# Old-state products, one chunk's scaling and the prologue's finishes of y in a fused attention and two-FFN kernel, put elsewhere

## The reference

```python
for t in range(S):
    cur = einsum('bhd,bhe->bhde', u[None] * kt, vt)
    y[:, :, t] = einsum('bhd,bhde->bhe', rt, state + cur)
    state = wt[:, :, :, None] * state + einsum('bhd,bhe->bhde', kt, vt)
x = y as (tokens, heads * channels)
h = x @ w_in;  x = where(h > 0, h, exp(min(h, 0)) - 1) @ w_out
out = sum over e of p[:, e:e+1] * (maximum(x @ w1[e], 0) @ w2[e])
```

## Time and profile before

| | |
|---|---|
| median of 3 runs | 698.22 us (696.87 to 699.43) |
| the profiled execution | 699.0 us, of which 696.8 are the span |
| TensorE matmuls busy | 99% of the span |
| VectorE busy | 38% |
| ScalarE busy | 26% |
| GpSimd busy | 23% |
| mean granted TensorE clock | 0.988 |

### The profile page before, as it was taken

One profiled execution on the slowest core, in us unless ns is written; L12 is line 12 of the kernel. 1 busy time (PEld: TensorE's weight loads), 2 busy tenths in 40 slices (PEclk: granted clock), 3 DMA queues, 4 the chain that ended last, 5 costly groups with the idle time before them and its releaser, 6 DMA issues.

```text
span 696.8 us, 10225 instructions
## 1 busy us (share of the span) xinstructions
PE 687.2 (99%) x3971; PEld 608.8 (87%) x3971; DVE 263.1 (38%) x471; ACT 181.3 (26%) x339; POOL 162.6 (23%) x181
## 2 busy tenths in 40 slices
PE   8989999999999999999999999999999999999998
PEld 6879999988878888899999999999999999999997
DVE  7568766675543433312131212121212121212122
ACT  3653443343343544411111111111111111111110
POOL 3899113110100366610005600006500000000000
PEclk9989999999999999999999999999999999999999
DMA  9902332220000232200002300003200000001011
GB/s 341 406 34 82 125 115 81 81 81 1 1 1 0 69 91 90 92 24 1 1 0 91 91 1 0 0 23 91 69 1 0 0 0 1 1 1 45 0 45 46
DMA packets 12854, 38.70 MB, mean 56 GB/s; under 512 B 1552, under 2 KB 3344, under 8 KB 12816
## 3 DMA queue, kind: packets, MB, share of 16 engines
q1 hardware_dynamic: 12528, 37.77, 15.9%
q10 hardware_dynamic: 288, 0.39, 0.2%
HBM read 35.80 MB, written 2.36 MB: 55 GB/s over the span
## 4 chain that ended last, share of the span: by engine, by line
PE 95%; DVE 3%; issue 1%; ACT 1%; DMA 0%; DVEq 0%
PE bank L852 29%; PE bank L854 29%; PE bank L853 28%; PE bank L804 3%; PE bank L760 2%; PE bank L800 1%; PE bank L815 1%; PE bank L771 1%; PE bank L784 1%; DVE w_lo L597 1%; DVE fr L514 1%; DVE bank L629 0%; DMA rkw<-rkw_dram 0%; PE bank L826 0%; DVE att L552 0%
## 5 line engine op out<-in xcount | busy, mean ns | idle before, releaser
L852 PE MATMUL bank<-x_lo,w_hi 128*128 128x512 f32 (+2 forms) x480 | 183.1, 382 | 1.2 <-DVE g_lo L635 0.9
L702 DVE SCALAR_TENSOR_TENSOR g_lo<-bank,g_hi 128x512 fp32r<-128x512 f32 x96 | 66.4, 691 | 308.5 <-ACT g_hi L482 308.5
L854 PE MATMUL bank<-x_hi,w_hi 128*128 128x512 f32 (+2 forms) x480 | 179.6, 374 | 0.0
L853 PE MATMUL bank<-x_hi,w_lo 128*128 128x512 f32 (+2 forms) x480 | 178.4, 372 | 0.0
L482 ACT ACTIVATE g_hi<-bank 128x512 fp32r<-128x512 f32 x96 | 57.5, 599 | 340.9 <-PE bank L854 340.9
L854 PE MATMUL bank<-w_hi,g_hi 128*128 128x384 f32 x384 | 129.7, 338 | 0.0
L853 PE MATMUL bank<-w_hi,g_lo 128*128 128x384 f32 x384 | 129.6, 337 | 0.0
L852 PE MATMUL bank<-w_lo,g_hi 128*128 128x384 f32 x384 | 129.3, 337 | 0.0
L854 PEld LDWEIGHTS bank<-x_hi,w_hi 128*128 128x128 f32 x480 | 91.1, 190 | 17.5
L852 PEld LDWEIGHTS bank<-x_lo,w_hi 128*128 128x128 f32 x480 | 91.1, 190 | 15.0 <-DVE g_lo L635 2.1
L853 PEld LDWEIGHTS bank<-x_hi,w_lo 128*128 128x128 f32 x480 | 91.4, 190 | 12.7
(11 more groups left out here) (67 smaller groups left out, 570.2 us busy)
## 6 DMA issues: line engine op xcount, KB each, us to landing
raw<-w_dram SPq DMA_DIRECT2D x48, 384.0 KB, 3.1
rkw<-rkw_dram SPq DMA_DIRECT2D x10, 772.5 KB, 4.4
tok<-tok_dram SPq DMA_DIRECT2D x12, 576.0 KB, 4.2
out_dram<-acc SPq DMA_DIRECT2D x10, 192.0 KB, 1.9
rkw<-rkw_dram SPq DMA_DIRECT2D x2, 512.0 KB, 4.5
rkw<-rkw_dram SPq DMA_DIRECT2D x2, 260.5 KB, 3.5
out_dram<-acc ACTq DMA_DIRECT2D x2, 192.0 KB, 1.9
u_rep<-u_dram SPq DMA_DIRECT2D x1, 192.0 KB, 6.2
```

The costliest lines, as they stand in the source:

```text
L702: dve.scalar_tensor_tensor(out=g2[1][:, r, :], in0=p_h[j % 2][:, :], scalar=0.0, in1=g2[0][:, r, :].bitcast(F32), op0=ALU.max, op1=ALU.sub ...
L852: pe.matmul(out, wh, ml, start=start, stop=False)
L853: pe.matmul(out, wl, mh, start=False, stop=False)
L854: return pe.matmul(out, wh, mh, start=False, stop=stop)
```

## The change

Four edits. `values` is cut in two: `old_values(c)` issues the sixteen products with the old state (and takes the waits for masks and state), and TensorE calls it two steps behind the scores, between `up(n)` and `down1(n - LAG)`; the products with the masked scores stay at the end of that step. The second half of the mask moves ahead of `elu`, next to the first. A second table, `SCALED`, equals `SCORES` but for chunk 2, whose entry is 6 instead of 7, and the scaling of k and r (`products`, `inverses`, `scale_k`, `scale_r`) follows it; `scale_state` does not. In the prologue, VectorE's second half of `lo_w(0)` goes behind both `finish_y`, and TensorE's single fill between the two turns of y goes behind them, to make four.

```diff
--- before.py
+++ after.py
@@ -65,6 +65,8 @@
 FIRST = TILES[0][1] // CH
 
 SCORES = {c: 4 * c - 1 for c in range(FIRST, NC)}
+
+SCALED = {c: step - (c == FIRST) for c, step in SCORES.items()}
 NUPDATE = NC - B
 LO_VECTOR = (0, 3, 5)
 LO_POOL = (1, 2, 4, 6, 7, 8, 9, 10, 11, 12, 13, 14, 15)
@@ -239,9 +241,9 @@
         def halves(ap):
             return ap.rearrange("p (a h i) -> p a h i", h=2, i=HALF)
 
-        def due(n, offset):
-
-            return [c for c, step in SCORES.items() if step + offset == n]
+        def due(n, offset, steps=SCORES):
+
+            return [c for c, step in steps.items() if step + offset == n]
 
         def rk_done(c):
             return 3 + 4 * (c - 1)
@@ -616,9 +618,9 @@
             mask_scores(1, 1, BANKS1)
             bonus(1)
             lo_w(0, 0)
-            lo_w(0, 1)
             finish_y(0, BANKS0)
             finish_y(1, BANKS1)
+            lo_w(0, 1)
             lo_x(0, BANKS0["yt"])
             lo_x(1, BANKS1["yt"])
 
@@ -659,6 +661,7 @@
             for n in range(STEP1):
                 for c in due(n, 1):
                     mask_scores(c, 0, BESIDE)
+                    mask_scores(c, 1, BESIDE)
                 for c in due(n, 3):
                     finish_y(c, BESIDE)
                 for c in due(n, 4):
@@ -668,8 +671,6 @@
                 elu(n)
                 for c in due(n, 0):
                     bonus(c)
-                for c in due(n, 1):
-                    mask_scores(c, 1, BESIDE)
                 for c in due(n, -1):
                     scale_state(c)
                 if n == 0:
@@ -685,12 +686,12 @@
                 if n in LO_AFTER:
                     lo_w(LO_AFTER[n], 0)
                     lo_w(LO_AFTER[n], 1)
-                for c in due(n, -3):
+                for c in due(n, -3, SCALED):
                     products(c)
-                for c in due(n, -2):
+                for c in due(n, -2, SCALED):
                     inverses(c)
                     scale_k(c)
-                for c in due(n, -1):
+                for c in due(n, -1, SCALED):
                     scale_r(c)
                 if n == STEP1 - J1 + 4:
                     normalise_probs()
@@ -786,23 +787,26 @@
                                         start=True, stop=True)
                 ins.then_inc(s_pu, 1)
 
+            def old_values(c, banks):
+
+                pe.wait_ge(s_att, c * 2 + 2)
+                pe.wait_ge(s_st, c - 1)
+                q = q_of(c)
+                for h in range(H):
+                    p, o = h // 2, h % 2
+                    rows = slice(64 * o, 64 * o + D)
+                    pe.matmul(banks["y"][o][:, p * D:(p + 1) * D], q[rows, p * CH:(p + 1) * CH],
+                              st[rows, c % 2, p, :], start=h < 2, stop=False, skip_group_check=True)
+
             def values(c, banks):
 
                 landed(pe, s_tok, c)
                 pe.wait_ge(s_att, c * 2 + 2)
-                q, v = q_of(c), v_of(c)
-                old = c >= FIRST
-                if old:
-                    pe.wait_ge(s_st, c - 1)
-                    for h in range(H):
-                        p, o = h // 2, h % 2
-                        rows = slice(64 * o, 64 * o + D)
-                        pe.matmul(banks["y"][o][:, p * D:(p + 1) * D], q[rows, p * CH:(p + 1) * CH],
-                                  st[rows, c % 2, p, :], start=h < 2, stop=False, skip_group_check=True)
+                v = v_of(c)
                 for h in range(H):
                     p, o = h // 2, h % 2
                     ins = pe.matmul(banks["y"][o][:, p * D:(p + 1) * D], att[:, o, p, :],
-                                    v[:, h * D:(h + 1) * D], start=not old and h == 0, stop=True,
+                                    v[:, h * D:(h + 1) * D], start=c < FIRST and h == 0, stop=True,
                                     skip_group_check=True)
                 ins.then_inc(s_py, 1)
 
@@ -841,9 +845,8 @@
             fill(1, 2)
             values(1, BANKS1)
             turn_y(0, BANKS0)
-            fill(1, 1)
             turn_y(1, BANKS1)
-            fill(3, 1)
+            fill(4, 1)
 
 
             def passes(out, w_parts, m_parts, start, stop):
@@ -897,6 +900,8 @@
                 if t == 0:
                     slice_ready(pe, j)
                 up(p_h[n % 2][:, 0:width(n)], tokens(t), j)
+                for c in due(n, 2):
+                    old_values(c, BESIDE)
                 if n >= LAG:
                     down1(n - LAG)
                 if n == 1:
```

## The result

Over eight runs the changed kernel has a median of 693.12 us (692.98 to 693.66), the kernel before 698.39 us (694.61 to 699.43) on the same chips: ratio 0.9934, 95% interval 0.9917 to 0.9952. That is 5.3 us less. As striking is the spread, 0.7 us against 4.8.

A forecast was written before the change was run, and what follows sets the result against it. TensorE, busy 687.2 of 696.8 us, was taken as the bound, with its stops and low clock. 0.75 + 2.2 + 2.96 - 1.6 = 4.3 off 699.0 gives 694.7, less 0.4 for run scatter: 694.3 us, range 692.4 to 697.3.

The forecast's parts named there:

- first rival: The stop ahead of step 7 brings no clock fall, full clock through step 7: 692.8 us, chance 0.28.
- The prologue: VectorE's second low half of slice 0 behind both finishes of y, first expansion sooner: 0.75 us won, bounds 0 and 1.0.
- The new stop: Chunk 2's earlier scaling: some 2.05 us stop ahead of step 7, short clock fall behind it; 2.2 us won.
- The split's gain: Old-state products between expansion and contraction: no clock falls behind the values, 2.96 us won, ends 0 and 2.96.
- The split's price: Extra change between wide and small matmuls, 0.16 us a chunk: 1.6 us lost over ten, ends 0 and 3.2.
- GpSimd: POOL's low parts of slices 13 to 15, slice 13 (near 58.2) needed at step 13: a little left, cost nothing.
- The sum: Whole kernel: 0.75 + 2.2 + 2.96 - 1.6 = 4.3 us won, 699.0 to 694.7, then 694.3 us.

The follow-up runs named there:

- unscaled_pool_b: pool_order with chunk 2's scaling back at its old steps; 693.57 us, ratio 0.9952.
- old_twice_b: The kernel before with the old-state products issued twice in a row; 711.59 us in two runs, ratio 1.0214.
- pool_order: The changed kernel with GpSimd's product of bonus and v of chunk 3 ahead of the low parts of slices 14 and 15; 691.79 us, ratio 0.9923.
- split_only: The kernel before with only the split of the values and the earlier second mask; 693.89 us, ratio 0.9954.
- scaled_only: The kernel before with only chunk 2's scaling a step earlier; 696.31 us, ratio 0.9987.
- no_split: The changed kernel with the old-state products back at the head of `values` and the second mask behind the ELU; 695.72 us, ratio 0.9981.
- one_step: The changed kernel with chunk 2's products in the same step as its inverses, lengthening the stop ahead of step 7; 694.51 us, ratio 0.9970.

## Why the prediction came out right, and which of its steps failed

The forecast was 694.3 us, the range 692.4 to 697.3, the measurement 693.12. The direction and the main cause were right; the gain was 5.3 us where 4.1 were forecast, and several terms missed in both directions. The measurement lies nearer to the first rival (692.8) than to the forecast.

- *The prologue*, 0.75: right, 0.88 at the first expansion between these two traces and 0.7 between the means of the others. By its times alone it could not be told from nothing.
- *The new stop.* That the 1.96 us delay would move to step 7, and TensorE's long wait turn from r's scaling to a low part, was right; the stop was 1.55 us, not 2.05. By the prediction's own numbers it should have been 0.28 + 1.96 = 2.24, so the 2.05 was not worked out from them. Two things made it shorter: inverses and scaling of k took 2.7 us (34.29 to 37.03 until the next ELU), not 3.05; and some of the delay already stood ahead of step 6, where TensorE was idle for 0.53 us. Together step 7 came 1.66 us late (38.37 against 37.59 - 0.88). A fall behind it was the step that failed: none came, in any of eight runs (mean clock 0.999 or 1.00). Step 9 starts 4.77 - 0.88 = 3.9 us sooner, where the forecast had 2.2. That is the first rival, given 0.28. The rule of the Trainium skill, page "TensorE: Matmul & The Clock Gate", section "HAM oscillation" is that the clock goes down when TensorE stands idle between bursts of matmuls for long enough. Of the stops here, 1.55 us without a fall and 3.4 us with one agree with it; 2.45 us and 2.3 us (unscaled_pool_b) with one do not, as these are shorter than it asks for. It doesn't cover falls at stretches of small products, of which old_twice_b shows six with TensorE never idle.
- *The split's gain*, 2.96: right, and shown three ways: alone it brings 3.3 us, without it the falls are back, and with the doubled products the clock falls six times unsplit and not once split. That the trace before had just two such falls was luck for the number: the runs of that kernel had mean clocks from 0.988 to 0.998.
- *The split's price*, 1.6: wrong, it is zero. The second block is 0.11 us shorter behind wide matmuls than behind small ones, which pays for the 0.10 us on the other side; why it is shorter is not shown. That was the lower end of the range given.
- *GpSimd*, "nothing": wrong, and the largest miss the other way, 1.66 us in steps 12 and 14. The prediction named it as what is late next, but took its times from the trace before, where it ended 2.27 us sooner, and weighed only slice 13 against step 13, and that from an even share (near 58.2; it ended at 59.13). The product of bonus and v behind slices 13 to 15 was not followed to the finish of y and the update. pool_order got 1.3 us of it back.
- *VectorE's finish of y in step 10*: no term. It cost 0.38 us, and pool_order, which does not touch it, still has 0.35.
- *The sum* came as near as it did because errors cancelled, which is luck: 1.7 us too little for the stop and its fall, 1.6 for the split's price, against 2.0 too much for the two waits that were put at nothing. In all 4.3 + 0.1 + 1.7 + 1.6 - 2.0 = 5.7 us, against 5.6 between the two profiled executions.

One thing the prediction did not see. Among the 35 runs of the kernel before beside split_only, those with a mean clock of 0.988 took about 699.1 us, of 0.993 about 697.2, of 0.998 about 694.6: some 1.1 us for each 0.0025, which is what one short fall takes off the mean (the traced run of scaled_only has one and 0.998). Carried on to 1.00 this gives about 693.5 us, an estimate; no run of it had a clock of 1.00. The changed kernel has 693.1, no_split without a fall 693.0, and split_only without one 692.95 to 693.62. So without falls the two kernels would be nearly equal: the time won by the scaling and the prologue went into the waits behind GpSimd and VectorE in steps 10 to 14, and what the change brings is nearly all the absence of falls.

Left open: why a stop of the same length brings a fall in one run and not in another. With a stop of 1.55 us none of eight runs had a mean clock below 0.999, with 2.4 us six of twelve had (split_only), with 2.3 us six of ten (unscaled_pool_b), with 3.4 us nine of ten (one_step); a fall behind the stop is seen in the one traced run of each, and some of the others may stand elsewhere, as in the prologue. Why GpSimd came later in the changed kernel is open as well. The doubled products without the split were timed in two runs only, one of them traced.

## What to carry to other kernels

On TensorE, look at the granted clock behind each long run of small products (here it was 0.50 to 0.65 over some 4 us behind some of them), and read it run by run: a spread of some us between runs can be falls that come or stay away. Breaking such a run with wide work that has to be done anyway costs nothing here and removed both the loss and the spread. When the bound engine is moved ahead, follow every other queue to each of its consumers, not only to the one that stands nearest, and don't count on the times of the old trace: here GpSimd's came 2.3 us later.

## What was not expected of the hardware

- The clock falls behind work in which TensorE is busy all the time: 2.84 us of small products without a break bring a fall behind some blocks (two of ten in the trace before, three in no_split), 3.7 us at six of ten, and pieces of 1.9 and 1.7 us with some 1.2 us of wide matmuls between them (more in the wider token tiles) at none.
- A change from wide matmuls to small ones and back in the middle of a step costs nothing in sum (5.06 us for the step both ways, and 0.02 us over the next eight such steps beside the two falls).
- The same program ran between 693.9 and 699.8 us on one chip, its time falling as the mean granted clock rises from 0.988 to 0.998.
